# Windowed attention and two gated MLPs on one core: the first four attention steps and the first weight casts in another order

## What is computed

```python
scores = scale * np.matmul(q, k.transpose(0, 1, 3, 2))
mask = (rel >= 0) & (rel < window)
...
return np.matmul(attn, v).astype(np.float32)
...
xn = x / rms * rms_g
g = xn @ w_gate
silu = g * (1.0 / (1.0 + np.exp(-g)))
val = xn @ w_val
return (silu * val @ w_out).astype(np.float32)
...
h = x @ w_in
g = h * (1.0 / (1.0 + np.exp(-1.702 * h)))
return (g @ w_out).astype(np.float32)
```

## Time and profile before

| | us |
|---|---|
| median of three executions | 904.75 |
| lowest, highest | 903.81, 905.58 |
| the profiled execution | 904.1 |
| its span, first to last instruction | 901.6 |
| PE busy | 889.1 |
| DVE busy | 539.6 |
| ACT busy | 398.5 |
| POOL busy | 82.2 |

### The profile page before, as it was taken

One profiled execution on the slowest core, in us unless ns is written; L12 is line 12 of the kernel. 1 busy time (PEld: TensorE's weight loads), 2 busy tenths in 40 slices (PEclk: granted clock), 3 DMA queues, 4 the chain that ended last, 5 costly groups with the idle time before them and its releaser, 6 DMA issues.

```text
span 901.6 us, 14706 instructions
## 1 busy us (share of the span) xinstructions
PE 889.1 (99%) x5372; PEld 771.3 (86%) x5372; DVE 539.6 (60%) x1256; ACT 398.5 (44%) x941; POOL 82.2 (9%) x114
## 2 busy tenths in 40 slices
PE   8899999999999999999999999999999999999998
PEld 7799888888888888888888899999999999999997
DVE  6886634334333343433336578887788788867663
ACT  5676333343333423334123354545464554545442
POOL 6234001030010300113000000000000000000000
PEclk9999999999999999999999999999999999999999
DMA  7672111102111021100500222121432122241201
GB/s 253 205 218 96 51 51 51 50 24 74 51 50 51 24 73 51 51 25 1 186 1 24 94 96 69 60 81 47 164 117 94 48 74 67 67 145 47 71 24 70
DMA packets 41078, 69.75 MB, mean 77 GB/s; under 512 B 3632, under 2 KB 13872, under 8 KB 41008
## 3 DMA queue, kind: packets, MB, share of 16 engines
q1 hardware_dynamic: 39600, 67.12, 23.0%
q10 hardware_dynamic: 1408, 1.70, 0.6%
HBM read 59.38 MB, written 9.44 MB: 76 GB/s over the span
## 4 chain that ended last, share of the span: by engine, by line
PE 94%; DVE 3%; ACT 2%; issue 1%; POOL 1%; POOLq 0%; ACTq 0%; DVEq 0%
PE ps L631 16%; PE ps L633 15%; PE ps L632 15%; PE ps L825 7%; PE ps L826 7%; PE ps L824 7%; PE ps L767 7%; PE ps L763 7%; PE ps L765 6%; PE ps L612 2%; PE ps L584 2%; PE ps L598 2%; DVE w_all L1197 1%; ACT prob L867 0%; DVE sig L1235 0%
## 5 line engine op out<-in xcount | busy, mean ns | idle before, releaser
L631 PE MATMUL ps<-x_hi,w_all 128*128 128x512 f32 (+1 forms) x480 | 179.4, 374 | 0.2 <-DVE x_lo L1137 0.2
L633 PE MATMUL ps<-x_lo,w_all 128*128 128x512 f32 (+1 forms) x480 | 176.7, 368 | 0.0
L632 PE MATMUL ps<-x_hi,w_all 128*128 128x512 f32 (+1 forms) x480 | 176.7, 368 | 0.0
L826 PE MATMUL ps<-w2out,hB 128*128 128x512 f32 x288 | 113.0, 392 | 0.0
L825 PE MATMUL ps<-w2out,hB 128*128 128x512 f32 x288 | 112.9, 392 | 0.0
L824 PE MATMUL ps<-w2out,hB 128*128 128x512 f32 x288 | 112.0, 389 | 0.0
L631 PEld LDWEIGHTS ps<-x_hi,w_all 128*128 128x128 f32 x480 | 90.4, 188 | 18.4 <-issue 3.0
L633 PEld LDWEIGHTS ps<-x_lo,w_all 128*128 128x128 f32 x480 | 90.4, 188 | 15.3
L632 PEld LDWEIGHTS ps<-x_hi,w_all 128*128 128x128 f32 x480 | 90.4, 188 | 14.6
L1235 DVE SCALAR_TENSOR_TENSOR sig<-sig,ps 128x512 f32<-128x512 f32 x48 | 32.9, 686 | 107.1 <-ACT sig L981 107.1
L631 PE MATMUL ps<-h_hi,w_all 128*128 128x512 f32 (+1 forms) x240 | 90.4, 376 | 1.8 <-DVE hid L1244 1.6
(11 more groups left out here) (144 smaller groups left out, 1557.0 us busy)
## 6 DMA issues: line engine op xcount, KB each, us to landing
wstage<-in_w_b SPq DMA_DIRECT2D x48, 512.0 KB, 3.7
wstage<-in_w_a SPq DMA_DIRECT2D x36, 256.0 KB, 3.2
vwin<-in_v_win SPq DMA_DIRECT2D x32, 256.0 KB, 3.9
kwin<-in_k_t SPq DMA_DIRECT2D x32, 160.0 KB, 3.3
x2raw<-x_scratch SPq DMA_DIRECT2D x3, 1536.0 KB, 7.5
out_dram<-yB SPq DMA_DIRECT2D x18, 256.0 KB, 4.4
qtok<-in_q_t SPq DMA_DIRECT2D x34, 128.0 KB, 2.6
x_scratch<-wstage SPq DMA_DIRECT2D x3, 1024.0 KB, 4.2
```

What stands on the lines that cost most here:

```text
L631: pe.matmul(out_, w[:, 0, cols], xh, start=first, stop=False, **flags)
L632: pe.matmul(out_, w[:, 1, cols], xh, start=False, stop=False, **flags)
L633: return pe.matmul(out_, w[:, 0, cols], xl, start=False, stop=last, **flags)
L826: ins = pe.matmul(y, hB_of(g, chunk, 1)[:, rows], w[:, 0, chunk, :], start=False, stop=last)
```

## The change

Low parts of the first three chunks get an order of their own (`FIRST_SPLITS`): (0,0), (0,1), (1,0), (1,1), (2,0), (0,2), (2,1), (1,2), (2,2). Casts of (0,1), (1,1), (2,0), (2,1) are ScalarE's; before, only (2,0) of the first three chunks was. On PE, transpose 2 goes ahead of v product 1 and transpose 3 ahead of v product 2, v product 3 ahead of `first_chunk_part(0)`, and two fill matmuls are gone. On ScalarE the four squares come behind all four `first_x_hi`. On DVE the reciprocal of step 3 comes ahead of the copy of the transposed block of step 1. The copies of steps 0 and 1 count on a semaphore of their own, `first_probT_ready`.

```diff
--- before.py
+++ after.py
@@ -202,6 +202,7 @@
         rec_order = sem("rec_order")
         probs_normed = sem("probs_normed")
         probs_transposed = sem("probs_transposed")
+        first_probT_ready = sem("first_probT_ready")
         probT_ready = sem("probT_ready")
         pv_done = sem("pv_done")
         o_evacuated = sem("o_evacuated")
@@ -254,20 +255,31 @@
             if value > 0:
                 eng.wait_ge(s, value)
 
+        def wait_probT(eng, n):
+            if n <= 2:
+                wait(eng, first_probT_ready, n)
+            else:
+                eng.wait_ge(probT_ready, n - 2)
+
         def slotA(c):
             return w_all[:, c * SLOT:(c + 1) * SLOT].rearrange("p (m s n) -> p m s n", m=3, s=2)
 
         def raw(u, m):
             return wstage[:, (3 * u + m) * DM:(3 * u + m + 1) * DM]
 
+        FIRST_SPLITS = ((0, 0), (0, 1), (1, 0), (1, 1), (2, 0), (0, 2), (2, 1), (1, 2), (2, 2))
+
         def splitsA(c, m):
-            return 3 * c + m + 1
+            return FIRST_SPLITS.index((c, m)) + 1 if c < 3 else 3 * c + m + 1
+
+        CASTS_BY_ACT = ((0, 1), (1, 1), (2, 0), (2, 1)) + tuple((c, m) for c in range(3, CA) for m in range(2))
+        CASTS_BY_POOL = ((0, 0), (1, 0), (0, 2), (1, 2)) + tuple((c, 2) for c in range(2, CA))
 
         def cast_by_act(c, m):
-            return (c, m) == (2, 0) or (c > 2 and m < 2)
+            return (c, m) in CASTS_BY_ACT
 
         def casts_so_far(by_act, c, m):
-            return sum(cast_by_act(*at_) == by_act for at_ in itertools.product(range(CA), range(3)) if at_ <= (c, m))
+            return (CASTS_BY_ACT if by_act else CASTS_BY_POOL).index((c, m)) + 1
 
         A11, A12, A22, S1, S2, S3, S4 = range(COMBOS)
         B11, B21, B22, T1, T2, T3, T4 = range(COMBOS)
@@ -534,16 +546,13 @@
             weights_hi_A(0, 0)
             normalise(1)
             normalise(2)
-            weights_hi_A(0, 1)
             normalise(3)
-            weights_hi_A(0, 2)
             weights_hi_A(1, 0)
             add_early_square(1)
-            weights_hi_A(1, 1)
-            weights_hi_A(1, 2)
+            weights_hi_A(0, 2)
             add_early_square(2)
             add_early_square(3)
-            weights_hi_A(2, 1)
+            weights_hi_A(1, 2)
             weights_hi_A(2, 2)
 
             for t in range(NA - 1):
@@ -574,7 +583,7 @@
                     pe.wait_ge(x_lo_ready, EARLY)
                     pe.wait_ge(ln_done, 1)
                 elif s % 2 == 0:
-                    pe.wait_ge(probT_ready, s)
+                    wait_probT(pe, s)
                     pe.wait_ge(ln_done, home_of(s)[0])
                 pe.wait_ge(qk_loaded[slot(s)], 32 * uses(s))
                 for m in range(GB // 2):
@@ -589,7 +598,7 @@
             def transpose_probs(s):
                 pe.wait_ge(probs_normed, s + 1)
                 if s < EARLY:
-                    wait(pe, probT_ready, s - 1)
+                    wait_probT(pe, s - 1)
                 else:
                     pe.wait_ge(max_ready, s - s % 2 + 2)
                 for h in range(2):
@@ -604,7 +613,7 @@
                 elif s >= EARLY and s % 2 == 0:
                     pe.wait_ge(hidA_made, chunk + 1 if chunk >= CA else chunk)
                 pe.wait_ge(v_loaded[slot(s)], 16 * uses(s))
-                pe.wait_ge(probT_ready, s + 1)
+                wait_probT(pe, s + 1)
                 for m in range(GB // 2):
                     for j in range(2):
                         for h in range(2):
@@ -618,7 +627,7 @@
                 n = TILES_A[t][1]
                 if t == 0:
                     pe.wait_ge(early_sums, EARLY - 1)
-                    pe.wait_ge(probT_ready, EARLY - 1)
+                    wait_probT(pe, EARLY - 1)
                     pe.matmul(ps[:, ATT_BANK, 0:n], ones[:, :], ss[:, 0:n], start=True,
                               stop=True).then_inc(sumsq_done, 1)
                     return
@@ -660,7 +669,7 @@
                 if t == 0 and c == 1:
                     pe.wait_ge(early_squares, 2)
                     pe.wait_ge(x_lo_ready, 2)
-                    pe.wait_ge(probT_ready, EARLY)
+                    wait_probT(pe, EARLY)
                 elif t == 0 and c == 2:
                     pe.wait_ge(early_squares, EARLY)
                     pe.wait_ge(x_lo_ready, EARLY)
@@ -719,15 +728,13 @@
             probs_by_v(0)
             transpose_probs(1)
             keep_busy(3, 2)
+            transpose_probs(2)
             probs_by_v(1)
-            transpose_probs(2)
+            transpose_probs(3)
             pe.wait_ge(max_ready, EARLY)
-            keep_busy(4, 2)
             probs_by_v(2)
-            transpose_probs(3)
-            first_chunk_part(0)
             probs_by_v(3)
-            for d in range(1, DC):
+            for d in range(DC):
                 first_chunk_part(d)
 
             for t in range(NA):
@@ -957,19 +964,20 @@
                 exponentials(s)
             act.wait_ge(g_loaded, 16)
             first_x_hi(0)
+            weights_hi_by_act(0, 1)
+            copy_probT(2)
             first_x_hi(1)
-            copy_probT(2)
-            first_square(0)
             copy_probT(3)
-            first_square(1)
             first_x_hi(2)
-            first_square(2)
             first_x_hi(3)
+            for s in range(EARLY):
+                first_square(s)
+            weights_hi_by_act(1, 1)
             nc.scalar.preload_act_table_set(LN_SET)
-            first_square(3)
             weights_hi_by_act(2, 0)
             act.wait_ge(consts_ready, 1)
             inverse_rms(0)
+            weights_hi_by_act(2, 1)
 
             def tanh_A(t, c):
                 n, w = CA * t + c, TILES_A[t][1]
@@ -1130,7 +1138,7 @@
 
             def evacuate_probT(s):
                 dve.wait_ge(probs_transposed, s + 1)
-                nc.vector.tensor_copy(probT_of(s), pt_of(s)).then_inc(probT_ready, 1)
+                nc.vector.tensor_copy(probT_of(s), pt_of(s)).then_inc(first_probT_ready, 1)
 
             def first_x_lo(s):
                 dve.wait_ge(x_hi_ready, s + 1)
@@ -1209,20 +1217,20 @@
             evacuate_probT(0)
             reciprocal_of_sum(2)
             weights_lo_A(0, 0)
+            reciprocal_of_sum(3)
             evacuate_probT(1)
-            reciprocal_of_sum(3)
             dve.wait_ge(g_loaded, 16)
             first_x_lo(0)
             weights_lo_A(0, 1)
             first_x_lo(1)
-            weights_lo_A(0, 2)
+            weights_lo_A(1, 0)
             first_x_lo(2)
-            weights_lo_A(1, 0)
             first_x_lo(3)
             weights_lo_A(1, 1)
+            weights_lo_A(2, 0)
+            weights_lo_A(0, 2)
+            weights_lo_A(2, 1)
             weights_lo_A(1, 2)
-            weights_lo_A(2, 0)
-            weights_lo_A(2, 1)
 
             def scale_gate(c):
                 dve.wait_ge(gate_done, c + 1)
```

## The result

Six executions of each: the changed kernel has a median of **908.84 us** (907.85 to 909.83), the kernel before 904.40 (903.81 to 905.58). The ratio is 1.0049 with a 95% interval of 1.0037 to 1.0061: slower by 4.4 us. The profiled execution took 908.07 us against 904.1, with a span of 906.1 instead of 901.6.

What follows compares the result with a forecast made beforehand. PE, busy 99%, was taken as the bound, with transpose 5's start deciding. Attention -1.2, cast +2.3 and held loads +1.5 gave +2.6 us: 906.7 for the profiled execution, 907.4 us as median, range 904.6 to 909.6.

Steps and rivals of the forecast that it cites:

- rival A: DMA landings repeat: (3,1) again lands 10 us behind (2,2), first product of chunk 1 +4.3 us, 909.1 us; chance 0.22.
- T, the issue of (2,2): Time SP may issue the load of (2,2), held for the sixth low part: 22.0 us, against 16.57 before.
- landing of (3,1) behind T: Load of (3,1) lands at T + 8.1, 30.1 us, one piece after the other, plus 0.2 us for remaining fetches.
- D, first product of chunk 1: Shift of DVE's first product of chunk 1, from 28.68 us, taken to shift transpose 5 equally: +2.6 us.
- from there to transpose 5: DVE works almost without pause from that product to transpose 5, so no further shift was expected: 0.
- the two bounds: Issue time of (2,2) by DVE's low parts: 21.6 us with two short ones, 22.4 with two of 1.0 us.
- The instruction fetch of 16 KB: Fetch at 23.0 us slowing DMA landings; follows PE's progress, so mostly gone from the new burst, 0.2 us left.
- The early gain of 1.2 us: Attention order on PE and DVE lets the sum of squares end at 21.4 instead of 22.57 us: -1.2 us.
- the two fills as 0.3 us: Two removed fill matmuls are about 0.3 us of PE that nobody waited for: 0 in the sum.
- -1.2, +2.3, +1.5: Attention order -1.2, cast behind the table load +2.3, loads behind (2,2) +1.5 us, added to +2.6.
- the cast behind the table load: ScalarE's cast of (2,1) behind its table load delays scale_gate(0) from 23.86 to 25.6 us: +2.3 us.
- Rival B: Quick landings, and PE's clock holds behind transpose 5, returning 1.3 us: shift -0.2 us, 904.6 us; chance 0.12.

Runs made afterwards that it cites:

- Run 4: Kernel before plus one wait: SP issues the load of (2,2) only after seven low parts; 907.32 us, ratio 1.0039.
- run 1: Changed kernel with q, k, v loads of steps 4 and 5 issued ahead of (2,2); 905.72 us, ratio 1.0022 to the kernel before.
- run 8: Run 5's kernel with the low part of (2,2) moved right behind scale_gate(0) on DVE; 903.19 us, ratio 0.9991 to the kernel before.
- Run 6: Kernel before with only the attention part of the change, casts and low-part order as before; 903.72 us, ratio 0.9999.
- run 5: Changed kernel with the edits of run 1 and run 2, plus cast and low part of (0,2) early; 903.24 us, ratio 0.9994 to the kernel before.
- run 2: Changed kernel with ScalarE's cast of (2,1) ahead of the inverse norm; 908.69 us, ratio 1.0052 to the kernel before.
- run 3: Changed kernel with q, k, v loads ahead of (2,2) and the cast of (2,1) ahead of the inverse norm; 904.45 us, ratio 1.0007 to the kernel before.
- Run 7: Kernel before with fill matmuls on PE, 2 ahead of transpose 4 and 7 between transposes 4 and 5; 903.57 us, ratio 0.9995.

## Why the prediction was right, and where its sum was off

**Direction and mechanism.** Slower was forecast with 0.64, at 907.4 us, in a range of 904.6 to 909.6. It was 908.84, nearest to rival A (909.1), but not by A's mechanism alone: (3,1) landed 9.1 us behind (2,2), half way between the forecast's 8.3 and A's 10.0. The steps named beforehand are all in the trace: SP's third piece held until the sixth low part, PE's wait for k, `scale_gate(0)` behind a cast behind a table load, ScalarE's wait for (3,0), and transpose 5 as the point where it counts. Run 4 shows the hold by itself to be worth 3.6 us, and run 1 that without it 2.0 are left.

**The sum**, +2.6 us forecast, +4.5 in the span of the profiled execution:

| term | forecast | measured | off by |
|---|---|---|---|
| T, the issue of (2,2) | 22.0 | 22.56 | +0.55 |
| landing of (3,1) behind T | 8.3 | 9.1 | +0.8 |
| D, first product of chunk 1 | +2.6 | +3.95 | +1.35 |
| from there to transpose 5 | 0 | +0.56 | +0.56 |

The sum was low by 1.8 us against the medians, 2.6 for 4.4, and all its errors point the same way. The number 907.4 looks closer, 1.4 off, by luck: it was built on 904.75, the median before of three executions, which is 904.40 with six.

T was near the upper one of the two bounds (22.4): both low parts ran beside POOL's cast. The port rule of the Trainium skill (Advanced Engine Details and Errata, GPSIMD Details) agrees with that, 1.94 us for two low parts beside a cast of POOL; what failed was the reading that three casts fewer would leave only short ones, 21.6. The landing was the mis-sized term. Pieces did land 0.6 to 0.7 us apart, but the v loads in front landed at 25.3 + 5.0 = 30.3, 7.7 us behind (2,2) where 6.7 was read from before. The instruction fetch of 16 KB, which I had blamed for 2 us, ran before the burst, as forecast, though not for the reason given, that it follows PE's progress: in run 4, with PE where it was before, it ran at 21.0 to 21.5 us instead of 23.0 to 23.5. The DMA queues of the changed kernel from 19.5 to 20.0 us (packets, MB, share of 16 engines):

```profile
q8 instruction: 1, 0.02, 12.5%
```

Still (3,0) needed 5.2 us from its issue instead of 6.2. So without that fetch the landing improved by 1 us and not by 2, and whether the fetch made even that 1 us is not shown. Smaller fetches of 8 KB, from queue q14, ran inside the burst too: two before, one after (27.0 to 27.5 us; another ran before its data moved), two in run 4, which landed soonest. No run shows the 0.2 us that the sum allowed for them. What makes the ninth DMA from (2,2) on, (3,1), land 8.4, 9.1 or 10.0 us behind its issue (run 4, after, before) stays open; no run separated it.

The last line of the table, which the forecast put at 0, goes by the trace alone. Four instructions of DVE between the product and transpose 5 took another time than before: the product itself 0.63 us instead of 0.41, the low part of (3,2) 1.10 instead of 0.69, the normalisation of step 4 1.04 instead of 0.69, each beside a cast of POOL, while the low part of (4,0), 1.10 before, took 0.68. Together that is the 0.56. POOL's casts in the changed kernel:

```profile
32.37 0.62 POOL L539 CAST w_all<-wstage 128x512 fp32r<-128x512 f32 x1 [5.90 <-DMA wstage<-in_w_a]
34.30 0.83 POOL L539 CAST w_all<-wstage 128x512 fp32r<-128x512 f32 x1 [1.31 <-DMA wstage<-in_w_a]
38.53 0.61 POOL L539 CAST w_all<-wstage 128x512 fp32r<-128x512 f32 x1 [3.40 <-DMA wstage<-in_w_a]
```

That the casts lengthen these instructions is read from their overlap, and run 8 shows it once more (1.10 us against 0.68 for the low part of (3,2)); no run moved the casts alone.

**The early gain of 1.2 us** was booked under attention. Run 6 shows it to be nothing there by itself. It came from attention and POOL's shorter list together, and the trace after shows 0.85 at the sum of squares; run 5 has 0.72 at transpose 5. The forecast had the second condition in its working (POOL's three adds and one cast) and not in its heading. Its reading of the two fills as 0.3 us of PE was low as well, 0.61 in the trace, without weight for the sum.

**The terms do not add.** I wrote -1.2, +2.3, +1.5 as a sum. Runs 1 to 3 show a maximum: the cast behind the table load is worth 0 us behind the hold (run 2) and 1.3 without it (run 1 against run 3). It was right to take the total at the landing, as the working did; the listing as three additive terms was not.

**Rival B and its 1.3 us.** The price of the fallen clock was wrong. It counted 12 slow matmuls and did not ask what PE does behind them: it waits for ScalarE's copies of the transposed blocks. PE's timeline shows the next v products, in the kernel before, and in run 3 with transpose 5 ahead of them:

```profile
53.27 1.18 PE L612 MATMUL ps<-probT,vwin 128*64 128x64 f32 x32 [0.25 <-ACT probT L894]
```

```profile
38.03 0.66 PE L608 MATMUL ps<-ident,prob 128*128 128x128 f32 x4 [1.45 <-DVE prob L1138]
...
53.56 1.17 PE L622 MATMUL ps<-probT,vwin 128*64 128x64 f32 x32 [0.73 <-ACT probT L902]
```

From transpose 5 to there it takes 15.63 us in the kernel before, with the fall (53.27 - 37.64), and 15.53 in run 3 (53.56 - 38.03), without it: the fall costs 0.1 us. With 0.1 in place of 1.3, B comes to 1.0 us above the kernel before and not below it. The executions of the kernel before in the set of runs 1 to 4 say the same: 11 with a mean granted clock of 1.00 have a mean span of 901.80 us, 12 with 0.998 have 901.85.

A longer fall does cost. In run 2 the clock was also down from before transpose 5, and in the windows from 42 to 48 us it stood at 0.50, where the changed kernel was back at 1.00 by 46 us. From transpose 5 (42.32) to the second of these v products it took 16.38 us, where the changed kernel, from 42.15, took 15.54:

```profile
45.93 1.98 PE L621 MATMUL ps<-probT,vwin 128*64 128x64 f32 x32
...
58.70 1.15 PE L621 MATMUL ps<-probT,vwin 128*64 128x64 f32 x32
```

```profile
57.69 1.17 PE L621 MATMUL ps<-probT,vwin 128*64 128x64 f32 x32
```

That is 0.84 us, and PE had no wait left there to hide it. The changed kernel's own executions may hold such a piece. Of its six, four have a mean granted clock of 0.994 and three of these a span of 907.1 or 907.2 us, while the two with 0.996 have 905.9 and 906.0. The profiled one, with 0.994, has 906.1; the others left no trace, so how much of the +4.4 is clock stays open, by these spans about 1 us at most. Run 7 also shows that transpose 5 itself is not the last link: 0.6 us later, it cost nothing. DVE's chain, on which both it and ScalarE's copies hang, is.

## What to carry to other kernels

When an order of work is changed and a semaphore counts that work, look for every wait on the count, also on engines that the diff does not touch: here DVE's new order delayed one DMA in SP's queue, and with it the eight behind it up to (3,1), on which tanh 1 hangs. Price such a hold by the first consumer of each queued load, and take the latest of the waits, not their sum. A stall or a slow clock is worth only what the next wait behind it does not take back (0.1 us of the fall in the kernel before, 0.84 of the longer one in run 2), so follow the engine to its next wait before putting a price on it.

## What the runs showed that was not expected

The fall of PE's clock does not follow the length of one gap. A gap of 2.17 us before transpose 5 brought it to 0.50 in the kernel before and not in run 5, where the window from 38 to 40 us has 1.00 behind the same 2.17:

```profile
38.00:40.00 2.00, 1.20 (x15) 1.02 (x15) 1.97 (x5) 1.23 (x3) 0.00 (x0) 1.00 0.71 176
```

In runs 1, 3 and 7 it fell one gap sooner, behind 3.92, 2.18 and 1.77 us before `project_A(0, 0)`, and then held at transpose 5; in the kernel before it had held behind 1.60 us there, and in run 6 behind 1.78, no shorter than run 7's 1.77. In the changed kernel and in run 2 it fell twice, in the wait for k and around transpose 5. The shorter falls have hardly a price of their own: from transpose 5 to the second v products behind it, the kernel before, the changed kernel and run 6, with a fall there, took 15.63, 15.54 and 15.51 us, and runs 1, 3, 4, 5 and 8, without one, 15.52 to 15.54. Run 2, with the longer fall, is the exception.
